# Retention, then two feed-forward layers, on one core: the first four chunks on two pairs of PSUM banks, with another order on VectorE and of the table loads

## The chip, the cores and the metric

The kernel runs on one core of a Trainium2 chip. The metric is the device time of one execution in microseconds (us), the median of several runs. One execution is also recorded by the hardware profiler; all views and rows below are of that one.

Engines, as the profile names them: PE is TensorE's matmul, PEld its weight load, DVE is VectorE, ACT is ScalarE, POOL is GpSimd, SP is SyncE, which issues most of the loads. Each engine runs its own instructions in order and waits for others by semaphores. A Q behind an engine's name (ACTq, SPq) is its sequencer, which issues DMAs.

## The reference

```python
def _attn_ref(q, k, v):                 # (4, 8, 768, 64) each
    gamma = 1.0 - 2.0 ** (-5.0 - np.arange(H, dtype=np.float32))
    for t in range(S):
        state = gamma[None, :, None, None] * state + np.einsum('bhd,bhe->bhde', k[:, :, t], v[:, :, t])
        y[:, :, t] = scale * np.einsum('bhd,bhde->bhe', q[:, :, t], state)

def _moe_ref(x, w_in, w_out):           # 3072 tokens, 512 -> 2048 -> 512
    h = x @ w_in
    g = np.where(h > 0.0, h, alpha * (np.exp(np.minimum(h, 0.0)) - 1.0))
    return g @ w_out

def _moe2_ref(x, w_in, w_out, g_ln):    # 512 -> 1024 -> 512
    h = x @ w_in
    sm = e / (np.sum(e, axis=-1, keepdims=True) + 1e-09)     # e = exp(h - max)
    solu = h * sm
    ln = (solu - mu) / np.sqrt(var + 1e-06) * g_ln
    return ln @ w_out
```

The three are chained: the output of the first, as 3072 tokens of 512 features, goes through the second and then the third.

## The kernel before

**Three stages.** The recurrence over time is done in chunks of C = 128 steps: 4 sequences of 6 chunks, 24 chunks, each with all 8 heads. Four chunks (CB = 4) make a block of 512 tokens, and there are NB = 6 blocks. Stage one turns chunks into attention outputs. Stage two is the feed-forward layer with 16 slices of 128 of its 2048 features per block: `up(j, f)` and `down(j, f)`. In it the chunks of the next block are worked in between, one per four slices. Stage three is the last layer, tile by tile of 128 tokens. All matrices are multiplied as a high and a low part, so each product is three matmuls, and ACT makes the high part and DVE the low part of everything.

**The opening.** This is where the change acts. Block 0 has no block before it to be worked into, so its four chunks run alone, ahead of `up(0, 0)`. For a chunk n the steps are:

- SP loads its tile in two halves of 512 KB (q and k transposed; then k and v). Before the others come the four small tables, which ACT issues: `v_decay` (4 KB), `q_decay` (256 KB), `causal` (64 KB), `state_decay` (2 KB).
- POOL: `decay_q(n)` (L326) multiplies q by `q_decay`, and `decay_v(n)` (L331) multiplies v by `v_decay`. It alternates the two, in the order of the chunks.
- TensorE: `scores(n)` (L394), 8 heads, fills two PSUM banks; it needs `decay_q(n)`. `key_values(n)` (L405) makes the chunk's addition to the state; it needs `decay_v(n)`. `values(n)` (L422 with the state, L425 with the masked scores) writes its output over the scores in the same two banks.
- DVE: `apply_mask(n)` (L589) copies the scores with the causal mask into `A[0]` or `A[1]` (A_68 and A_69 in the instruction lists below). `update_state(n)` (L610, or L613 and L615) makes the next state.
- `attended(n)`: ACT copies the output out of the banks as the high part `x_hi` (L776, semaphore `att_hi`), and then DVE subtracts this from the banks' content for the low part `x_lo` (L594, semaphore `att_lo`). After that the chunk's banks are free.

**Banks.** `att_bank(n)` gives the first of the two banks of a chunk. In the opening it is 2, 0, 4, 2 for chunks 0 to 3. Later chunks all have bank 2. The banks 6 and 7 belong to `key_values`. In stage two banks 0 and 1 are for `up`, 4 to 7 for `down`.

**What sets the order.** It is written out by hand for each engine. TensorE: `scores(0)`, then per chunk `key_values(n)`, `scores(n + 1)`, `values(n)` (L485 to L496). `scores(3)` waits for `att_lo` 1 (L383), since it takes chunk 0's banks. ACT alternates `attended(n)` and `split_hi`, which makes the high part of a block of weights; DVE's list in L622 to L641 has `split_lo` for their low parts among its chunk steps. `up(0, 0)` (L440, L441, then L446) starts when `att_hi` says that all four chunks have their high part. Ahead of `scores(0)` there are 14 matmuls on a tile of zeros (L484), which keep TensorE at work while the first tile is loaded.

Of the kernel before, what the change touches and what calls it, by code (L numbers as in the profile page):

```python
# [6 lines left out]
B, H, S, D = 4, 8, 768, 64  # L7
# [13 lines left out]
CB = TB // C  # L21
# [11 lines left out]
def build(nc, units, w1, w_in2, w_out2, g_ln, tables, x2_dram, out):  # L33
# [4 lines left out]
    with ctx:  # L38
# [31 lines left out]
        v_decay = place("v_decay", H, f32, CONST_AT + 32)  # L70
# [48 lines left out]
        ps = ctx.enter_context(nc.psum_tensor("ps", [P, 8 * 512], f32))[:, :].rearrange("p (b c) -> p b c", c=512)  # L119

        def att_bank(n):
            return (2, 0, 4, 2)[n] if n < CB else 2

        def ps_scores(n, h):
            return ps[:, att_bank(n) + h // HH, (h % HH) * C:(h % HH + 1) * C]
# [94 lines left out]
        def up_count(f):  # L220
            return 2 * f + 1
# [157 lines left out]
        def _(pe):  # L379

            def scores(n):
                pe.wait_ge(q_decayed, n + 1)
                if n == CB - 1:  # L383

                    pe.wait_ge(att_lo, 1)
                if n >= CB:

                    pe.wait_ge(att_lo, n)
                    pe.wait_ge(state_done, states(n))
                qt, kt = tile_of(n)[:, QT], tile_of(n)[:, KT]  # L390
                for hh in range(HH):
                    for h in (hh, HH + hh):
                        c = slice(hh * C, hh * C + C)
                        last = nc.tensor.matmul(ps_scores(n, h), kt[rows(h), c], qt[rows(h), c], start=True, stop=True)  # L394
                last.then_inc(scores_done, 1)

            def key_values(n):
                pe.wait_ge(v_decayed, n + 1)
                if 2 <= n < CB:
                    pe.wait_ge(state_done, states(n - 1))  # L400
                k, v = tile_of(n)[:, KN], tile_of(n)[:, VN]
                for hh in range(HH):
                    for h in (hh, HH + hh):
                        one = slice(h * D, (h + 1) * D)
                        last = nc.tensor.matmul(ps_kv(n)[rows(h), hh, :], k[:, one], v[:, one], start=True, stop=True,  # L405
                                                skip_group_check=True)
                last.then_inc(kv_done, 1)

            def values(n):
                c = n % NC  # L410
                qt, v = tile_of(n)[:, QT], tile_of(n)[:, VN]
                masked_scores = A[1 if n < CB and n % 2 else 0]
                pe.wait_ge(masked, n + 1)
                pe.wait_ge(v_decayed, n + 1)
                if c > 0:
                    pe.wait_ge(state_done, states(n))
                    for pair in range(2):
                        for half in range(2):
                            for odd in range(2):
                                h = HH * half + 2 * pair + odd  # L420
                                hh = h % HH
                                nc.tensor.matmul(ps_y(n, h), state[rows(h), n % 2, hh, :], qt[rows(h), hh * C:hh * C + C],  # L422
                                                 start=(pair == 0), stop=False, skip_group_check=True)
                for h in range(H):
                    last = nc.tensor.matmul(ps_y(n, h), v[:, h * D:(h + 1) * D], masked_scores[:, h, :],  # L425
                                            start=(c == 0 and h % HH < 2), stop=True, skip_group_check=True)
                last.then_inc(chunk_done, 1)
# [55 lines left out]
            for _ in range(WARM):  # L483
                nc.tensor.matmul(ps[:, 7, :], warm[:, 0:P], warm[:, :], start=True, stop=True)  # L484
            scores(0)  # L485
            key_values(0)
            scores(1)
            values(0)
            key_values(1)
            scores(2)  # L490
            values(1)
            key_values(2)
            scores(3)
            values(2)
            key_values(3)
            values(3)  # L496

            for j in range(NB):
                up(j, 0)
# [79 lines left out]
        def _(dve):  # L579

            def apply_mask(n):
                dve.wait_ge(scores_done, n + 1)
                before = n - 2 if n < CB else n - 1
                if before >= 0:

                    dve.wait_ge(chunk_done, before + 1)
                out_ = A[1 if n < CB and n % 2 else 0]
                scored = ps[:, att_bank(n):att_bank(n) + 2, :].rearrange("p b (h t) -> p (b h) t", h=HH)
                nc.vector.tensor_tensor(out_, scored, causal[:, :].unsqueeze(1).to_broadcast([P, H, C]), ALU.mult)\  # L589
                    .then_inc(masked, 1)  # L590

            def attended(n):
                dve.wait_ge(att_hi, n + 1)
                nc.vector.tensor_tensor(block_cols(x_lo, n), ps_y_all(n), block_cols(x_hi, n).bitcast(f32), ALU.subtract)\  # L594
                    .then_inc(att_lo, 1)

            def update_state(n):
                if n % NC == NC - 1:
                    return
                dve.wait_ge(kv_done, states(n + 1))  # L600
                if n > 0:

                    dve.wait_ge(chunk_done, n)
                if n >= CB:

                    dve.wait_ge(att_hi, n + 1)
                old, new = state[:, n % 2, :, :], state[:, (n + 1) % 2, :, :]
                decay = state_decay[:, :].unsqueeze(2).to_broadcast([P, HH, D])
                if n % NC == 0:
                    nc.vector.tensor_tensor(new, ps_kv(n), decay, ALU.mult).then_inc(state_done, 1)  # L610
                else:
                    dve.wait_ge(state_done, states(n))
                    nc.vector.tensor_tensor(state_sum, ps_kv(n), old, ALU.add).then_inc(state_summed, 1)  # L613
                    dve.wait_ge(state_summed, n - 2 * (n // NC))
                    nc.vector.tensor_tensor(new, state_sum, decay, ALU.mult).then_inc(state_done, 1)  # L615

            def split_lo(n, count):
                dve.wait_ge(w_hi_done, count)
                nc.vector.tensor_tensor(w_lo[:, n, :], w_raw[:, n, :], w_hi[:, n, :].bitcast(f32), ALU.subtract)\
                    .then_inc(w_lo_done, 1)  # L620
# [3 lines left out]
            dve.wait_ge(state_decay_in, 16)  # L624
            update_state(0)
            apply_mask(1)
            update_state(1)
            attended(0)
            apply_mask(2)
            update_state(2)  # L630
            apply_mask(3)
            attended(1)
            split_lo(0, up_count(0))
            attended(2)
            attended(3)
            split_lo(NF1, down_count(0))
# [118 lines left out]
        def _(act):  # L755
            for one_up in (y_sb_done, y_out[0], y_out[1]):
                act.sem_inc(one_up, 1)

            act.dma_start(v_decay[:, :], tables[:, T_VDEC:T_VDEC + H]).then_inc(v_decay_in, 16)
            act.dma_start(q_decay[:, :], tables[:, T_QDEC:T_QDEC + HH * C]).then_inc(q_decay_in, 16)  # L760
            act.dma_start(causal[:, :], tables[:, T_CAUSAL:T_CAUSAL + C]).then_inc(causal_in, 16)
            act.dma_start(state_decay[:, :], tables[:, T_SDEC:T_SDEC + HH]).then_inc(state_decay_in, 16)

            def split_hi(n):
# [170 lines left out]
```

## Time and profile before

| what | value |
|---|---|
| time, median of 3 runs | 904.7 us (904.67 to 904.89) |
| time of the profiled execution | 904.89 us |
| its span in the trace | 903.1 us |
| TensorE matmul busy | 894.6 us (99%) |
| VectorE / ScalarE / GpSimd busy | 408.0 / 304.1 / 117.3 us |
| mean granted clock of TensorE | 0.998 of full |
| HBM read / written | 44.44 / 12.58 MB |

The span is the time from the first to the last recorded instruction; the execution's own time is 1.79 us longer. A matmul's end is modelled, so two neighbouring ones overlap in the list: the distance of their starts tells the rate. The granted clock is the share of full speed that TensorE was allowed. In the rows below a bracket such as `[0.70 <-ACT x_hi L776]` says how long the engine was idle before the instruction and what ended that.

### The profile page before, as it was taken

The page shows a single profiled execution, that of the slowest core. Times are in us where ns is not written, and L with a number is a line of the kernel's source. Part 1 is how long each engine was busy: PE and PEld are TensorE (multiplying, and loading weights), DVE is VectorE, ACT ScalarE, POOL GpSimd, SP SyncE. Part 2 cuts the span into 40 slices and gives each one's busy share as a digit, 9 for nine tenths or more (in the row PEclk, how much of TensorE's full clock was granted, in tenths as well). Part 3 has the DMA queues.
Part 4 walks back from the last instruction along what each step waited for, and adds up shares of the span by engine and source line. Part 5 has one row for each costly group of instructions (what it writes and reads, how often), then busy time and mean ns, then how long its engine had stood idle before and what let it go on. Part 6 is the DMA issues. An engine that isn't in the chain of part 4 may idle for free.

```text
span 903.1 us, 12782 instructions
## 1 busy us (share of the span) xinstructions
PE 894.6 (99%) x5070; PEld 732.0 (81%) x5070; DVE 408.0 (45%) x712; ACT 304.1 (34%) x509; POOL 117.3 (13%) x106
## 2 busy tenths in 40 slices
PE   8999999999999999999999999999999999999998
PEld 6788888888888888888888888887888888888887
DVE  4765533332323333333423332266765655566563
ACT  2645332322423233332423333353232223322322
POOL 4211101110201111110200000122211111111110
PEclk9999999999999999999999999999999999999999
DMA  9901131110410131110400020312111111111100
GB/s 349 406 18 40 47 94 47 48 48 1 140 32 16 47 94 47 47 47 1 140 1 1 1 70 1 120 63 75 43 38 35 46 46 46 46 46 46 46 35 36
DMA packets 33675, 57.65 MB, mean 64 GB/s; under 512 B 3040, under 2 KB 15584, under 8 KB 33632
## 3 DMA queue, kind: packets, MB, share of 16 engines
q1 hardware_dynamic: 33056, 56.70, 18.2%
q8 instruction: 32, 0.52, 0.2%
q10 hardware_dynamic: 576, 0.33, 0.1%
q14 instruction: 11, 0.09, 0.0%
HBM read 44.44 MB, written 12.58 MB: 63 GB/s over the span
## 4 chain that ended last, share of the span: by engine, by line
PE 96%; DVE 1%; issue 1%; POOL 0%; DMA 0%; ACT 0%; DVEq 0%; POOLq 0%; ACTq 0%
PE ps L462 11%; PE ps L466 10%; PE ps L463 10%; PE ps L440 10%; PE ps L441 10%; PE ps L446 10%; PE ps L535 5%; PE ps L537 5%; PE ps L536 5%; PE ps L477 4%; PE ps L479 4%; PE ps L478 4%; PE ps L394 3%; PE ps L425 3%; PE ps L523 2%
## 5 line engine op out<-in xcount | busy, mean ns | idle before, releaser
L462 PE MATMUL ps<-g_hi,w_hi 128*128 128x512 f32 x384 | 154.0, 401 | 0.0
L651 DVE TENSOR_TENSOR g_lo<-e,g_hi 128x512 fp32r<-128x512 f32 x96 | 74.9, 780 | 170.3 <-ACT g_hi L803 170.1
L440 PE MATMUL ps<-x_hi,w_hi 128*128 128x512 f32 x384 | 149.5, 389 | 0.7 <-ACT x_hi L776 0.7
L466 PE MATMUL ps<-g_lo,w_hi 128*128 128x512 f32 x384 | 149.9, 390 | 0.0
L463 PE MATMUL ps<-g_hi,w_lo 128*128 128x512 f32 x384 | 149.6, 390 | 0.0
L441 PE MATMUL ps<-x_hi,w_lo 128*128 128x512 f32 x384 | 149.4, 389 | 0.0
L646 DVE SCALAR_TENSOR_TENSOR e<-e,ps 128x512 f32<-128x512 f32 x96 | 65.7, 684 | 141.0 <-ACT e L797 141.0
L803 ACT ACTIVATE g_hi<-e 128x512 fp32r<-128x512 f32 x96 | 60.7, 632 | 198.4 <-PE ps L466 187.1
L795 ACT ACTIVATE e<-ps 128x512 f32<-128x512 f32 x96 | 57.3, 597 | 149.6 <-PE ps L446 148.8
L446 PE MATMUL ps<-x_lo,w_hi 128*128 128x512 f32 x384 | 102.6, 389 | 0.0
L462 PEld LDWEIGHTS ps<-g_hi,w_hi 128*128 128x128 f32 x384 | 72.0, 188 | 17.9 <-issue 0.7
L440 PEld LDWEIGHTS ps<-x_hi,w_hi 128*128 128x128 f32 x384 | 72.1, 188 | 15.9 <-ACT x_hi L776 0.9
L466 PEld LDWEIGHTS ps<-g_lo,w_hi 128*128 128x128 f32 x384 | 72.1, 188 | 15.4
L441 PEld LDWEIGHTS ps<-x_hi,w_lo 128*128 128x128 f32 x384 | 72.1, 188 | 15.0
L446 PEld LDWEIGHTS ps<-x_lo,w_hi 128*128 128x128 f32 x384 | 72.1, 188 | 15.0
L463 PEld LDWEIGHTS ps<-g_hi,w_lo 128*128 128x128 f32 x384 | 72.1, 188 | 14.0
L326 POOL TENSOR_TENSOR tiles<-tiles,q_decay 128x512 f32<-128x512 f32 x23 | 31.8, 1384 | 385.9 <-DMA tiles<-units_dram 379.5
L535 PE MATMUL ps<-w_hi,n_hi 128*128 128x512 f32 x192 | 75.0, 391 | 0.1
L537 PE MATMUL ps<-w_hi,n_lo 128*128 128x512 f32 x192 | 74.9, 390 | 0.0
L536 PE MATMUL ps<-w_lo,n_hi 128*128 128x512 f32 x192 | 74.7, 389 | 0.0
L477 PE MATMUL ps<-w_hi,x_hi 128*128 128x512 f32 x184 | 73.7, 400 | 0.0
L479 PE MATMUL ps<-w_hi,x_lo 128*128 128x512 f32 x184 | 71.8, 390 | 0.0
(82 smaller groups left out, 1067.8 us busy)
## 6 DMA issues: line engine op xcount, KB each, us to landing
tiles<-units_dram SPq DMA_DIRECT2D x46, 512.0 KB, 4.7
w_raw<-w_dram SPq DMA_DIRECT2D x32, 256.0 KB, 9.5
x_between<-x SPq DMA_DIRECT2D x24, 256.0 KB, 2.7
x_tile<-x_between SPq DMA_DIRECT2D x24, 256.0 KB, 2.7
out_dram<-y_sb SPq DMA_DIRECT2D x24, 256.0 KB, 2.0
w_raw<-w_in_dram SPq DMA_DIRECT2D x4, 512.0 KB, 5.0
w_raw<-w_out_dram SPq DMA_DIRECT2D x4, 512.0 KB, 3.4
tile<-units_dram SPq DMA_DIRECT2D x2, 512.0 KB, 10.1
```

Source lines behind the costliest of these rows:

```text
L440: nc.tensor.matmul(bank, hi, x_hi[:, j % 2, k, :], start=(k == 0), stop=False)
L441: nc.tensor.matmul(bank, lo, x_hi[:, j % 2, k, :], start=False, stop=False)
L446: last = nc.tensor.matmul(bank, hi, x_lo[:, j % 2, k, :], start=False, stop=(k == KD - 1))
L462: nc.tensor.matmul(ps[:, 4 + m, :], hi, g_hi[:, f % 2, :], start=(f == 0), stop=False)
L463: nc.tensor.matmul(ps[:, 4 + m, :], lo, g_hi[:, f % 2, :], start=False, stop=False)
L466: last = nc.tensor.matmul(ps[:, 4 + m, :], hi, g_lo[:, f % 2, :], start=False, stop=(f == NF1 - 1))
L477: nc.tensor.matmul(bank, x_h[:, k, :], hi, start=(k == 0), stop=False)
L479: last = nc.tensor.matmul(bank, x_l[:, k, :], hi, start=False, stop=(k == KD - 1))
L535: nc.tensor.matmul(bank, n_hi[:, par, f, :], hi, start=(f == 0), stop=False)
L536: nc.tensor.matmul(bank, n_hi[:, par, f, :], lo, start=False, stop=False)
L537: last = nc.tensor.matmul(bank, n_lo[:, par, f, :], hi, start=False, stop=(f == NF2 - 1))
L651: nc.vector.tensor_tensor(g_lo[:, f % 2, :], e[:, f % 2, :], g_hi[:, f % 2, :].bitcast(f32), ALU.subtract)\
```

## The change

Four edits, all of them in the opening. (1) The chunks 0 to 3 have the bank pairs 2, 4, 2, 4 in place of 2, 0, 4, 2, so in the opening each chunk takes the pair of the chunk two before. Therefore `scores(2)` and `scores(3)` wait until `att_lo` has 1 and 2. (2) The TensorE order of the opening is written as a loop. (3) On DVE `attended(0)` goes ahead of `update_state(1)`, and `attended(1)` and `split_lo(0)` go ahead of `update_state(2)` and `apply_mask(3)`. (4) ACT issues the table `v_decay` third in place of first.

```diff
@@ -119,7 +119,7 @@
         ps = ctx.enter_context(nc.psum_tensor("ps", [P, 8 * 512], f32))[:, :].rearrange("p (b c) -> p b c", c=512)
 
         def att_bank(n):
-            return (2, 0, 4, 2)[n] if n < CB else 2
+            return 4 if n < CB and n % 2 else 2
 
         def ps_scores(n, h):
             return ps[:, att_bank(n) + h // HH, (h % HH) * C:(h % HH + 1) * C]
@@ -380,12 +380,11 @@
 
             def scores(n):
                 pe.wait_ge(q_decayed, n + 1)
-                if n == CB - 1:
-
-                    pe.wait_ge(att_lo, 1)
+                before = n - 2 if n < CB else n - 1
+                if before >= 0:
+
+                    pe.wait_ge(att_lo, before + 1)
                 if n >= CB:
-
-                    pe.wait_ge(att_lo, n)
                     pe.wait_ge(state_done, states(n))
                 qt, kt = tile_of(n)[:, QT], tile_of(n)[:, KT]
                 for hh in range(HH):
@@ -483,17 +482,11 @@
             for _ in range(WARM):
                 nc.tensor.matmul(ps[:, 7, :], warm[:, 0:P], warm[:, :], start=True, stop=True)
             scores(0)
-            key_values(0)
-            scores(1)
-            values(0)
-            key_values(1)
-            scores(2)
-            values(1)
-            key_values(2)
-            scores(3)
-            values(2)
-            key_values(3)
-            values(3)
+            for n in range(CB):
+                key_values(n)
+                if n + 1 < CB:
+                    scores(n + 1)
+                values(n)
 
             for j in range(NB):
                 up(j, 0)
@@ -624,13 +617,13 @@
             dve.wait_ge(state_decay_in, 16)
             update_state(0)
             apply_mask(1)
+            attended(0)
             update_state(1)
-            attended(0)
             apply_mask(2)
+            attended(1)
+            split_lo(0, up_count(0))
             update_state(2)
             apply_mask(3)
-            attended(1)
-            split_lo(0, up_count(0))
             attended(2)
             attended(3)
             split_lo(NF1, down_count(0))
@@ -756,9 +749,9 @@
             for one_up in (y_sb_done, y_out[0], y_out[1]):
                 act.sem_inc(one_up, 1)
 
-            act.dma_start(v_decay[:, :], tables[:, T_VDEC:T_VDEC + H]).then_inc(v_decay_in, 16)
             act.dma_start(q_decay[:, :], tables[:, T_QDEC:T_QDEC + HH * C]).then_inc(q_decay_in, 16)
             act.dma_start(causal[:, :], tables[:, T_CAUSAL:T_CAUSAL + C]).then_inc(causal_in, 16)
+            act.dma_start(v_decay[:, :], tables[:, T_VDEC:T_VDEC + H]).then_inc(v_decay_in, 16)
             act.dma_start(state_decay[:, :], tables[:, T_SDEC:T_SDEC + HH]).then_inc(state_decay_in, 16)
 
             def split_hi(n):
```

TensorE in the opening, from `key_values(1)` on, before and then after. The names in it: `tiles` and `tile_67` are the chunks' inputs, `ps` is PSUM.

```order
L405 MATMUL ps<-tiles 64x64 [waits v_decayed]
L405 MATMUL ps<-tiles 64x64 x7
L394 MATMUL ps<-tiles 128x128 [waits q_decayed]
L394 MATMUL ps<-tiles 128x128 x7
L422 MATMUL ps<-tiles,state 64x128 [waits state_done,v_decayed,masked]
```

```order
L404 MATMUL ps<-tiles 64x64 [waits v_decayed]
L404 MATMUL ps<-tiles 64x64 x7
L393 MATMUL ps<-tiles 128x128 [waits att_lo,q_decayed]
L393 MATMUL ps<-tiles 128x128 x7
L421 MATMUL ps<-tiles,state 64x128 [waits state_done,v_decayed,masked]
```

Nothing has moved on TensorE; `scores(2)` has a second wait, `att_lo`. The lines of the changed kernel have other numbers (one lower here, seven lower on DVE and ACT). `scores(3)` has that wait in both, for a higher count after.

DVE in the opening, from the mask of chunk 1 to the mask of chunk 3, before and then after:

```order
L589 TENSOR_TENSOR A_69<-ps,causal 128x1024 [waits scores_done]
L613 TENSOR_TENSOR state_sum<-ps,state 128x256 [waits state_done,chunk_done,kv_done]
L615 TENSOR_TENSOR state<-state_sum,state_decay 128x256 [waits state_summed]
L594 TENSOR_TENSOR x_lo<-ps,x_hi 128x4x128 [waits att_hi]
L589 TENSOR_TENSOR A_68<-ps,causal 128x1024 [waits chunk_done,scores_done]
L613 TENSOR_TENSOR state_sum<-ps,state 128x256 [waits state_done,chunk_done,kv_done]
L615 TENSOR_TENSOR state<-state_sum,state_decay 128x256 [waits state_summed]
L589 TENSOR_TENSOR A_69<-ps,causal 128x1024 [waits chunk_done,scores_done]
```

```order
L582 TENSOR_TENSOR A_69<-ps,causal 128x1024 [waits scores_done]
L587 TENSOR_TENSOR x_lo<-ps,x_hi 128x4x128 [waits att_hi]
L606 TENSOR_TENSOR state_sum<-ps,state 128x256 [waits state_done,chunk_done,kv_done]
L608 TENSOR_TENSOR state<-state_sum,state_decay 128x256 [waits state_summed]
L582 TENSOR_TENSOR A_68<-ps,causal 128x1024 [waits chunk_done,scores_done]
L587 TENSOR_TENSOR x_lo<-ps,x_hi 128x4x128 [waits att_hi]
L612 TENSOR_TENSOR w_lo<-w_raw,w_hi 128x512 [waits w_hi_done]
L606 TENSOR_TENSOR state_sum<-ps,state 128x256 [waits state_done,chunk_done,kv_done]
L608 TENSOR_TENSOR state<-state_sum,state_decay 128x256 [waits state_summed]
L582 TENSOR_TENSOR A_69<-ps,causal 128x1024 [waits chunk_done,scores_done]
```

The subtraction `x_lo` of chunk 0 now stands ahead of the two steps of the state of chunk 1, and that of chunk 1 together with the first `w_lo` ahead of those of chunk 2.

ACT's first four instructions that issue DMAs, before and then after, with what follows them:

```order
L759 DMA v_decay<-tables_dram 128x8
L760 DMA q_decay<-tables_dram 128x512
L761 DMA causal<-tables_dram 128x128
L762 DMA state_decay<-tables_dram 128x4
L776 ACT_TABLE_LOAD
```

```order
L752 DMA q_decay<-tables_dram 128x512
L753 DMA causal<-tables_dram 128x128
L754 DMA v_decay<-tables_dram 128x8
L755 DMA state_decay<-tables_dram 128x4
L769 ACT_TABLE_LOAD
```

`v_decay` has moved from the first to the third place of the queue.

## Rows read from the trace of the kernel before

**Rows 1.** The page, part 4: shares of the chain that ended last, by engine.

```profile
PE 96%; DVE 1%; issue 1%; POOL 0%; DMA 0%; ACT 0%; DVEq 0%; POOLq 0%; ACTq 0%
```

**Rows 2.** The chain of the first 30 us: start us, duration us, what.

```profile
13.34 1.02 PE ps L425 x16
...
17.54 0.46 PE ps L405 x16
...
21.78 1.05 PE ps L425 x16
...
22.85 0.61 ACT x_hi L776
```

**Rows 3.** Timeline of TensorE: start us, duration us, work [idle before it].

```profile
8.95 1.49 PE L394 MATMUL ps<-tiles 64*128 64x128 f32 x16 [2.03 <-POOL tiles L326]
...
11.42 1.92 PE L394 MATMUL ps<-tiles 64*128 64x128 f32 x16
13.27 1.09 PE L425 MATMUL ps<-A,tiles 128*64 128x128 f32 x16
...
14.76 1.16 PE L394 MATMUL ps<-tiles 64*128 64x128 f32 x16
15.85 0.67 PE L422 MATMUL ps<-tiles,state 64*64 64x128 f32 x16
...
17.93 1.16 PE L394 MATMUL ps<-tile 64*128 64x128 f32 x16
...
23.50 0.50 PE L440 MATMUL ps<-x_hi,w_hi 128*128 128x512 f32 x1 [0.70 <-ACT x_hi L776]
23.84 0.40 PE L441 MATMUL ps<-x_hi,w_lo 128*128 128x512 f32 x1
24.08 0.40 PE L440 MATMUL ps<-x_hi,w_hi 128*128 128x512 f32 x1
```

**Rows 4.** Timeline of VectorE, opening.

```profile
13.39 1.23 DVE L589 TENSOR_TENSOR A<-ps,causal 128x1024 f32<-128x1024 f32 x1 [1.28 <-PE ps L394]
...
23.48 0.69 DVE L594 TENSOR_TENSOR x_lo<-ps,x_hi 128x512 fp32r<-128x512 f32 x1 [1.32 <-ACT x_hi L776]
```

**Rows 5.** Timeline of all engines, start: when four loads are issued.

```profile
0.96 0.39 ACTq L759 DMA_DIRECT2D v_decay<-tables_dram  x1
...
1.39 0.45 ACTq L760 DMA_DIRECT2D q_decay<-tables_dram  x1
1.67 0.43 SPq L236 DMA_DIRECT2D tiles<-units_dram  x1
...
1.86 0.45 ACTq L761 DMA_DIRECT2D causal<-tables_dram  x1
```

**Rows 6.** DMA issues: KB each, us from issue to landing.

```profile
q_decay<-tables_dram ACTq DMA_DIRECT2D x1, 256.0 KB, 6.2
causal<-tables_dram ACTq DMA_DIRECT2D x1, 64.0 KB, 7.3
...
v_decay<-tables_dram ACTq DMA_DIRECT2D x1, 4.0 KB, 4.1
...
tiles<-units_dram SPq DMA_DIRECT2D x1, 512.0 KB, 7.0
```

**Rows 7.** Timeline of GpSimd, opening.

```profile
7.63 1.26 POOL L326 TENSOR_TENSOR tiles<-tiles,q_decay 128x512 f32<-128x512 f32 x1 [6.33 <-DMA q_decay<-tables_dram]
8.85 1.05 POOL L331 TENSOR_TENSOR tiles<-tiles,v_decay 128x512 f32<-128x512 f32 x1
9.85 1.27 POOL L326 TENSOR_TENSOR tiles<-tiles,q_decay 128x512 f32<-128x512 f32 x1
```

**Rows 8.** Stretches: busy us (PE, PEld, DVE, ACT, POOL), clock, DMA share, GB/s.

```profile
9.00:9.50 0.50, 0.50 (x9) 0.50 (x11) 0.00 (x0) 0.00 (x0) 0.50 (x1) 1.00 1.06 321
...
10.00:13.00 3.00, 3.00 (x35) 2.66 (x34) 1.56 (x2) 0.00 (x0) 3.00 (x3) 0.50 1.02 399
...
13.50:20.00 6.50, 6.50 (x134) 5.78 (x132) 5.87 (x8) 2.23 (x4) 3.32 (x3) 1.00 1.04 407
```

## The prediction, made before the changed kernel ran

> **What bounds the kernel now.** I read the page's chain first: 96% of what ended last is TensorE [rows 1]. So only time that TensorE loses counts, and I ask where the edits touch its path. They all act in the opening, the four chunks of block 0 before the first `up`. Next, the chain of the first 30 us: chunk 0's `values` ends at 13.34 + 1.02 = 14.36 us, chunk 1's at 17.54 us, where L405 begins, chunk 3's at 21.78 + 1.05 = 22.83 us, and the first `up` waits for ACT's copy of it [rows 2]. The timeline of TensorE has two idle times from 7 us on: 2.03 us for the first decayed q, and 0.70 us before `up` [rows 3]. Between them a next group is ready at once: TensorE is the bound there too. Behind `up(0, 0)` at 23.50 us no edit follows, and TensorE is the chain, so a later `up(0, 0)` moves the end by the same amount. The weights go on loading by SP's own order, and a later TensorE gives them more time.
>
> The profiled execution is 904.89 us (span 903.1 and 1.79 around it); the median of the three runs is 904.70. I work out a difference and put it on the median.
>
> **The banks and the new waits (a cost).** Before, chunks 1 and 2 have banks of their own: `scores(2)` starts at 14.76 us, right behind `key_values(1)`, and `scores(3)` at 17.93 us right behind `key_values(2)` [rows 3]. With two pairs, `scores(2)` needs the pair of chunk 0, which is free when both `attended` of chunk 0 have read it. The path from the end of a `values` to there, from chunk 3, whose copy and subtraction have no other work ahead of them: chain end 22.83, ACT L776 from 22.85, DVE L594 from 23.48 for 0.69, ends 24.17 [rows 2, 4]. With 0.04 from there to a matmul (as from ACT's end at 22.85 + 0.61 = 23.46 to 23.50 [rows 2, 3]) that is 24.21 - 22.83 = 1.38 us. Under it lies only `key_values(1)`, which filled what was a 0.40 us step from 14.36 to 14.76 [rows 2, 3]. Stall one: 1.38 - 0.40 = 0.98 us. For `scores(3)`, which before waited only for chunk 0's `att_lo`, long there: 17.93 - 17.54 = 0.39, so stall two is 0.99 us. A restart costs a little more: at 23.50 us the first step from matmul to matmul is 0.34 us, the next 0.24 [rows 3], so 0.10 each, 0.20. Sum 2.17 us, or 1.97 if the 64-row matmuls restart free.
>
> **The DVE order.** `attended(0)` now stands ahead of `update_state(1)`, and `attended(1)` and the first `split_lo` ahead of `update_state(2)`. Without this the stalls would be longer. Is DVE free for `attended(0)`? The mask of chunk 1 starts 0.05 us behind the scores (13.39 to 13.34) and lasts 1.23 [rows 2, 4]; the scores' end plus `values(0)` (1.02) plus ACT's copy (0.65) is later, at 1.67. Yes, by 0.39 us. What is queued behind: `update_state(1)` needs two operations half as wide as L594's, at most 0.69 us each, while `values(2)`, which wants that state, is over 3 us away. `mask(3)` waits behind `attended(1)`, `split_lo(0)` and `update_state(2)`. Counted from the end of `scores(1)`, `attended(1)` ends at about 6.6 us (the two stalls and 1.62 us per `values` laid end to end); three operations of at most 0.69 and the mask's 1.23 end by 9.9, and `values(3)` wants the mask at 9.8 to 9.9. So the cover is small but there even at that upper bound: the edit costs nothing, 0.1 us at worst. The loop in place of the written-out list issues the same TensorE groups in the same order: 0.
>
> **The table loads (both signs).** On ACT's queue the first three tables landed in order: `v_decay` 0.96 + 4.1 = 5.06, `q_decay` 1.39 + 6.2 = 7.59, `causal` 1.86 + 7.3 = 9.16 [rows 5, 6]. The sizes are 4, 256 and 64 KB, yet the steps behind the first are 2.5 and 1.6 us: each costs its place among SP's 512 KB loads more than its bytes. If the first 256 KB take the first place, `q_decay` lands about 1 us (2.5 less the 1.6 of a place) behind 5.06, at 6.1 (5.1 to 7.2), not 7.6. But `v_decay` is now third, and the first three together still end near 9.16 (8.6 to 9.6): I take that row, since the three transfers are the same. GpSimd runs in order: `decay_q(0)` 6.1 to 7.4, then it waits until 9.2 for the 4 KB table, `decay_v(0)` 1.05 to 10.25, `decay_q(1)` 1.27 to 11.52 [rows 7]. So `scores(0)` starts 1.5 us earlier, at 7.45, and `key_values(0)` near 10.3, but `scores(1)` near 11.58: 0.16 us later than the 11.42 of before [rows 3]. What was a gain at the head is given back behind it. The `causal` table lands earlier than now and its mask is not near it.
>
> The Trainium skill, page "DMA: Bandwidth & Descriptors", section "Anatomy of one DMA", gives a fixed cost of about 2.0 us for a transfer plus its bytes at 436 GB/s (measured there on GpSimd's path). By it 4 KB issued at 1.86 us would be there at 3.9 us and GpSimd would never wait for it; that is the rival N below. The trace doesn't agree: 4.1 us for the same 4 KB at the head of its queue, and 7.3 us for 64 KB in third place [rows 6].
>
> **The clock.** The granted clock is full (2.4 GHz) up to 9.5 us, half (1.2 GHz) from 10 to 13 us, and full again from 13.5 us [rows 8]. It fell after TensorE had stood for 2.03 us and worked again for about 0.6 us [rows 3], and rose after it had worked without a gap. At half level lay `key_values(0)` and nearly all of `scores(1)`, whose step to `values(0)` is 13.27 - 11.42 = 1.85 us against 1.09 for the same group at 14.76 (to 15.85) [rows 3]. In the changed kernel TensorE has done 1.1 us more by then but again stands for about 1.8 us and 0.8 us. I cannot compute what the chip decides. I take the low stretch as it was (in `scores(1)`), because TensorE is still idle for most of the time between 6.9 and 11.6 us. Then `values(0)` starts at 13.27 + 0.16.
>
> **Sum.** 0.16 + 0.98 + 0.99 + 0.20 = 2.33 us over the median: 907.0 us. A measurement of this kernel can tell about 0.2%, 1.8 us, from no change: the bounds are 902.9 and 906.5.
>
> **Rivals.**
> H, the clock holds: enough work comes early that it never falls. `scores(1)` takes 1.09, `values(0)` starts at 12.67, 0.60 us earlier than now; -0.60 + 2.17 = +1.57, 906.3 us. For it: `scores(0)` at 7.45 follows the warm-up after 0.5 us. Against: the gap just moves behind `scores(0)`.
> L, the clock stays low longer, or falls later and covers `values(0)`, `key_values(1)` and part of `scores(2)`. At half level the 1.02 and 0.46 us of the first two double: +1.5 us, less what the stall hides of it. With the front as in H that comes to about 907.2, with the front as forecast to about 908.3. For it: the two stalls put idle time into what was an unbroken stretch.
> N, `v_decay` isn't late (the other side, not slower). If it lands by 7.4 us, GpSimd goes on at once: `decay_v(0)` to 8.45, `decay_q(1)` when its tile is there (1.67 + 7.0 = 8.7 [rows 5, 6]), to about 10.12. `scores(1)` starts at 10.17, 1.25 us earlier than now, and with a full clock ends 2.01 us earlier; against 2.17 of stalls that is 904.9 us, no difference. With a low clock it is 905.9. It decides below a landing of 8.1 us or so, from which point the front gains more than 0.5 us. Against it: the landings in order of issue.
> F, faster by more than 1.8 us: N, and both stalls hidden. Nothing covers them on TensorE.
>
> **How the numbers follow.** Forecast as worked out, with the milder form of L (906.7 to 907.5): 0.46. H 0.23. Harder L (907.9 to 908.6) 0.14. N 0.14, mostly 904.9 to 905.9. F 0.03. Slower by over 0.2%: nearly all of the forecast (0.43), all of the harder L (0.14), a quarter of H (0.06): 0.63. Faster 0.03. Same 0.34. The range, which leaves out half of N, the upper half of L's hard form and F, is 905.4 to 908.3; with 0.1 to 0.4 us for the cover of `mask(3)` and the landing of `v_decay` it needs no more.
>
> **What would show it.** Right: TensorE stands for about 1 us ahead of `scores(2)` and again ahead of `scores(3)`, each ended by DVE's `x_lo`; GpSimd stands between `decay_q(0)` and `decay_v(0)`, ended by `v_decay`; `scores(0)` near 7.5 us; the first `up` near 25.8 us; from there on the same distances as now. Wrong: stalls under 0.5 us each (then DVE or ACT is quicker than chunk 3's rows say); GpSimd going on at once (N); a granted clock without the low stretch (H) or with a longer one (L); or a wait named behind the first `up` that wasn't there. The forecast is wrong in sign if the first `up` starts before 23.5 us.

## The result, and the profile after

| | before | changed |
|---|---|---|
| median, 5 runs each | 904.7 us (904.41 to 904.89) | 909.56 us (908.45 to 910.17) |
| ratio, 95% interval | | 1.0055 (1.0044 to 1.0067) |
| profiled execution, its span | 904.89, 903.1 us | 909.62, 907.8 us |

The changed kernel is slower by 4.9 us, where 2.3 were forecast: the direction was right, and the time lies above the range. The five executions spread over 1.7 us, those of before over 0.5; in 14 executions in all the changed kernel took 908.39 to 911.29 us.

The chain of the first 34 us of the changed kernel (start, duration, what) answers to [rows 2]:

```profile
9.83 1.04 POOL tiles L331
...
12.15 1.42 PE ps L393 x16
13.57 1.93 PE ps L424 x16
...
15.52 0.61 ACT x_hi L769
...
16.15 0.70 DVE x_lo L587
...
16.98 1.16 PE ps L393 x16
...
21.05 1.63 DVE w_lo L612
...
23.40 1.23 DVE A L582
...
30.37 2.65 DVE w_lo L612 x3
...
33.67 0.50 PE ps L439
```

Read it against the prediction. The chain no longer starts at a q: it comes over `decay_v(0)` on GpSimd (L331), which waits for `v_decay`. `scores(1)` (L393) starts at 12.15 us, `values(0)` (L424) at 13.57 takes 1.93 us, and then the two stalls come as forecast: ACT's `x_hi`, DVE's `x_lo`, the next `scores` at 16.98 and again at 21.28. New is that between the second stall and the first `up` (27.06 us) a weight subtraction on DVE (L612, 1.63 us) and the mask it holds up (L582) are on the chain; and behind the first `up` DVE is on it once more, until the third `up` (L439) starts at 33.67 us. By engine, the page says of the whole chain, against [rows 1], 94% in place of 96% for TensorE and 2% in place of 1% for VectorE:

```profile
PE 94%; DVE 2%; issue 1%; DMA 1%; POOL 1%; ACT 0%; ACTq 0%; DVEq 0%; POOLq 0%
```

TensorE's waits from 6 to 60 us (total, times, longest):

```profile
PE ps L404 <- POOL tiles L331: 2.2, 1, 2.2
PE ps L393 <- DVE x_lo L587: 1.7, 2, 1.1
...
PE ps L439 <- DVE e L639: 0.9, 1, 0.9
PE ps L439 <- ACT x_hi L769: 0.7, 1, 0.7
```

The last but one of these isn't in the kernel before: 0.88 us for DVE's `e`, behind the first `up`. The third `up` (`up(0, 2)`) starts here in the kernel before (TensorE, timeline):

```profile
29.11 0.39 PE L440 MATMUL ps<-x_hi,w_hi 128*128 128x512 f32 x1
```

and here in the changed one:

```profile
33.67 0.50 PE L439 MATMUL ps<-x_hi,w_hi 128*128 128x512 f32 x1 [0.88 <-DVE e L639]
```

From the first `up` to the third it is 29.11 - 23.50 = 5.61 us before ([rows 3] for the first) and 33.67 - 27.06 = 6.61 after. With that the loss of the profiled execution can be cut up along TensorE's starts in the timeline (where `values(0)` starts at 13.50, a little ahead of the chain's 13.57):

| step | before | after | later by |
|---|---|---|---|
| to `values(0)` | 13.27 | 13.50 | 0.23 |
| `values(0)` to `scores(2)` | 1.49 | 3.48 | 1.99 |
| `scores(2)` to `scores(3)` | 3.17 | 4.30 | 1.13 |
| `scores(3)` to the first `up` | 5.57 | 5.78 | 0.21 |
| first `up` to third | 5.61 | 6.61 | 1.00 |

The sum is 4.56 of the 4.73 us between the two profiled executions. The second row holds the first stall (0.66 us of idle time, ended by DVE's `x_lo`) and the slow clock of `values(0)` and `key_values(1)`; the third holds the second stall, 1.05 us idle.

Two of the tables (KB, us from issue to landing) answer to [rows 6]; they are issued at 0.96 and 1.87 us:

```profile
q_decay<-tables_dram ACTq DMA_DIRECT2D x1, 256.0 KB, 5.3
...
v_decay<-tables_dram ACTq DMA_DIRECT2D x1, 4.0 KB, 7.9
```

`q_decay` lands at about 6.25, `v_decay` at about 9.76 us, in third place. And the granted clock, with the columns of [rows 8]:

```profile
9.00:12.50 3.50, 1.04 (x22) 0.90 (x24) 1.54 (x2) 0.00 (x0) 2.67 (x3) 1.00 1.00 347
13.00:16.00 3.00, 3.00 (x36) 2.78 (x36) 1.22 (x1) 0.48 (x1) 3.00 (x4) 0.50 1.03 416
17.00:20.00 3.00, 3.00 (x62) 2.71 (x64) 2.04 (x3) 0.19 (x1) 0.56 (x1) 1.00 1.05 417
```

It is full until 12.5 us, half from 13 to 16 us and full again. The low stretch lies about 3 us later than in before, over `values(0)` and `key_values(1)` instead of `key_values(0)` and `scores(1)`.

### The profile page after: what moved, and what is told of

Same layout as the page of the kernel before. It is cut to its first block, busy times and chain, and to the rows that moved or that the text cites. A ratio compares the mean times of both kernels' runs of the same rounds, so it can differ in the third digit from the quotient of the medians.

```text
span 907.8 us, 12783 instructions
## 1 busy us (share of the span) xinstructions
PE 895.2 (99%) x5070; PEld 732.0 (81%) x5070; DVE 410.8 (45%) x712; ACT 304.0 (33%) x509; POOL 115.8 (13%) x106
## 4 chain that ended last, share of the span: by engine, by line
PE 94%; DVE 2%; issue 1%; DMA 1%; POOL 1%; ACT 0%; ACTq 0%; DVEq 0%; POOLq 0%
PE ps L461 11%; PE ps L465 10%; PE ps L462 10%; PE ps L439 9%; PE ps L440 9%; PE ps L445 9%; PE ps L528 5%; PE ps L530 5%; PE ps L529 5%; PE ps L476 4%; PE ps L478 4%; PE ps L477 4%; PE ps L424 3%; PE ps L393 3%; PE ps L516 2%; PE ps L421 1%
## 5 line engine op out<-in xcount | busy, mean ns | idle before, releaser
L439 PE MATMUL ps<-x_hi,w_hi 128*128 128x512 f32 x384 | 149.6, 390 | 1.6 <-DVE e L639 0.9
L439 PEld LDWEIGHTS ps<-x_hi,w_hi 128*128 128x128 f32 x384 | 72.1, 188 | 17.1 <-DVE e L639 1.3
```

The costliest lines, as they stand in the source:

```text
L439: nc.tensor.matmul(bank, hi, x_hi[:, j % 2, k, :], start=(k == 0), stop=False)
```

## The experiments

Three letters name the parts of the change: B is the two bank pairs with their waits, D the order on VectorE, T the table order. B can't be had with the old order on VectorE, since there `attended(1)` stands behind `mask(3)`, which would then wait for it in a circle. The executions of one kernel differ in their mean granted clock; where an execution is said to be at full clock, that mean is 0.999 or 1.000. Where a profile was taken, the low stretch lies in the opening. Before, at full clock, lies at 903.8 to 904.5 us (904.1 in the middle), at 0.998 at 904.4 to 905.2; one execution at 0.996 took 908.26.

**D alone**, `D_order_only`:

```diff
-            update_state(1)
             attended(0)
+            update_state(1)
             apply_mask(2)
-            update_state(2)
-            apply_mask(3)
             attended(1)
             split_lo(0, up_count(0))
+            update_state(2)
+            apply_mask(3)
```

> The kernel before with the new VectorE order alone (banks and tables as before). Theory A (the parts add up from waits in the opening): attended(0) goes ahead of the state of chunk 1, nothing on TensorE waits for either early, so 904.7 us, within 0.3. Rival B (the order itself costs, because update_state(2) and mask(3) stand behind a weight subtraction): first up later by 0.3 to 1 us, 905.0 to 905.7.

Measured: 905.11 us against 904.43, ratio 1.0002 (0.9991 to 1.0012); at full clock 904.14 to 904.56, else 905.0 to 906.2. No difference that the interval tells, though the trace has a small one. TensorE, and then DVE:

```profile
21.52 0.67 PE L422 MATMUL ps<-tile,state 64*64 64x128 f32 x16 [0.31 <-DVE A L589]
```

```profile
18.85 0.68 DVE L619 TENSOR_TENSOR w_lo<-w_raw,w_hi 128x512 fp32r<-128x512 f32 x1
...
20.25 1.22 DVE L589 TENSOR_TENSOR A<-ps,causal 128x1024 f32<-128x1024 f32 x1
```

`mask(3)` (L589) starts at 20.25 us, behind the subtraction at 18.85 and the state, though its scores ended at about 19.1; so `values(3)` starts at 21.52, 0.31 us after TensorE could have gone on. The prediction had worked out the cover for the changed kernel, where the stalls give VectorE more time; here there are none, so this wait doesn't contradict it.

**T alone**, `T_tables_only`, and **D and T without B**, `DT_banks_back`:

```diff
-            act.dma_start(v_decay[:, :], tables[:, T_VDEC:T_VDEC + H]).then_inc(v_decay_in, 16)
             act.dma_start(q_decay[:, :], ...)
             act.dma_start(causal[:, :], ...)
+            act.dma_start(v_decay[:, :], tables[:, T_VDEC:T_VDEC + H]).then_inc(v_decay_in, 16)
```

> The kernel before with v_decay issued third and nothing else. Theory A: v_decay lands near 9.76 us as in the changed kernel, scores(1) starts near 12.15 instead of 11.42; the granted clock then falls later and lies over values(0) and key_values(1): first up 0.7 to 1.6 us later than 23.5, and 905.4 to 906.5 in all, with runs that differ by up to 2 us according to where the low stretch falls. Rival B (most of the loss is the tables and the clock): 907 or more. Rival C (only the banks cost): 904.7.

> The changed kernel with the four banks of before back (chunks 1 and 2 on their own pairs), new VectorE order and new table order kept. Theory A: the two stalls ahead of scores(2) and scores(3) are gone, first up near 24.6 to 25.1, no wait for VectorE behind it: 905.5 to 906.7. Rival B (tables and clock carry the loss): over 907.5.

Measured: T 906.82 us (904.47 to 908.99), ratio 1.0024 (1.0011 to 1.0037). DT 907.26 us (906.75 to 909.51), ratio 1.0038 (1.0024 to 1.0052). Both medians lie between theory A and rival B, above what the waits in the opening add up to. T's ten executions fall into groups: 904.47 to 904.77 at full clock, 905.4 to 906.9 at 0.998, 908.4 to 909.0 at 0.996. So moving one 4 KB table costs 0.4 to over 4 us in the same program, and the time follows the clock. The profiled execution of T (908.42 us, clock 0.996) shows how a low clock comes to cost so much. Its first `up` starts at 25.44 us, 1.94 us later than before. Its third starts here:

```profile
32.52 0.50 PE L440 MATMUL ps<-x_hi,w_hi 128*128 128x512 f32 x1 [1.35 <-DVE e L646]
```

That is 7.08 us behind the first, 1.47 more than before, although T changes nothing on VectorE and adds no bank wait. The two parts, 3.41 us, are nearly all of the 3.53 us between the two executions. DT has the same in small: 1.55 us by the first `up`, and 6.23 us from there to the third. What the second part is comes below.

**B and D without T**, `BD_v_first`, the changed kernel with `v_decay` first:

> The changed kernel with v_decay issued first again; two bank pairs and new VectorE order kept. Theory A: GpSimd does not wait, scores(1) at 11.42 as before, two stalls of 1.0 to 1.1 us, first up near 25.7; behind it VectorE's weight subtractions meet GpSimd's decays of chunks 4 and 5 and run longer, up(0, 2) waits up to 0.9 us: 906.9 to 907.9. Rival B (tables and clock carry the loss): under 906.2.

Measured: 907.82 us (906.58 to 909.02), ratio 1.0039 (1.0026 to 1.0051); three executions at full clock took 906.6 to 907.0, three at 0.998 took 908.7 to 909.0. The profiled execution was at full clock, and shows the stalls clean (TensorE, timeline):

```profile
13.23 0.64 PE L404 MATMUL ps<-tiles 128*64 128x64 f32 x16
14.91 1.16 PE L393 MATMUL ps<-tiles 64*128 64x128 f32 x16 [1.05 <-DVE x_lo L587]
...
17.53 0.63 PE L404 MATMUL ps<-tiles 128*64 128x64 f32 x16
19.21 1.16 PE L393 MATMUL ps<-tile 64*128 64x128 f32 x16 [1.05 <-DVE x_lo L587]
...
24.78 0.50 PE L439 MATMUL ps<-x_hi,w_hi 128*128 128x512 f32 x1 [0.70 <-ACT x_hi L769]
...
31.02 0.50 PE L439 MATMUL ps<-x_hi,w_hi 128*128 128x512 f32 x1 [0.50 <-DVE e L639]
```

From the start of `key_values` (L404) to the next `scores` it is 1.68 us both times, against 0.57 us for the same step before (14.19 to 14.76 us): 1.11 us each, of which the rows name 1.05 as idle. These are the two stalls of the forecast. The first `up` comes at 24.78 us. But the third comes 6.24 us behind it, with an idle 0.50 us for DVE, where `D_order_only` (23.91 to 29.50) has 5.59.

**Why does DVE come late?** In this part of the changed kernel the weight subtractions (L612) that last longer than 0.68 us (one) or 1.89 us (three in a row) lie beside GpSimd's decays of chunks 4 and 5:

```profile
21.05 1.63 DVE L612 TENSOR_TENSOR w_lo<-w_raw,w_hi 128x512 fp32r<-128x512 f32 x1
...
30.29 2.73 DVE L612 TENSOR_TENSOR w_lo<-w_raw,w_hi 128x512 fp32r<-128x512 f32 x3
```

```profile
20.87 1.26 POOL L326 TENSOR_TENSOR tiles<-tiles,q_decay 128x512 f32<-128x512 f32 x1 [3.31 <-DMA tiles<-units_dram]
...
28.48 1.60 POOL L326 TENSOR_TENSOR tiles<-tiles,q_decay 128x512 f32<-128x512 f32 x1 [3.98 <-DMA tiles<-units_dram]
30.05 1.22 POOL L331 TENSOR_TENSOR tiles<-tiles,v_decay 128x512 f32<-128x512 f32 x1
```

The subtraction from 21.05 lasts 1.63 us; GpSimd's decay runs from 20.87 to 22.13, and 22.13 plus 0.55 is the subtraction's end. This is what the Trainium skill, page "SBUF — State Buffer", section "SBUF: two separate sides", describes: VectorE with two SBUF inputs and GpSimd take a shared port pair in turn, whoever starts first for its whole instruction. The end 0.55 us behind the decay agrees with that. The trace alone doesn't prove it, since the weight loads run then too. Two experiments take the meeting away. `BDT_small_45` is the changed kernel with almost nothing for GpSimd to do in those chunks:

```diff
+                w = 1 if n in (4, 5) else HH * C
-                nc.gpsimd.tensor_tensor(qt, qt, q_decay[:, :], ALU.mult).then_inc(q_decayed, 1)
+                nc.gpsimd.tensor_tensor(qt[:, 0:w], qt[:, 0:w], q_decay[:, 0:w], ALU.mult).then_inc(q_decayed, 1)
```

(and `decay_v` likewise, to one column of each head).

> The changed kernel in which GpSimd's decays of chunks 4 and 5 work on one column in place of all (this leaves out part of the decay of these two chunks), so that they last 0.1 to 0.2 us each. Theory A (VectorE's subtractions with two inputs in SBUF stand while a GpSimd decay runs, and this lengthens the way to up(0, 2)): the 1.63 us subtraction ahead of mask(3) takes 0.7, the three ahead of the first elu take 1.9 in place of 2.7, no wait for VectorE ahead of up(0, 2); 0.9 to 1.4 us less than the changed kernel: 908.1 to 908.7 where that has 909.5. Rival B (VectorE is late by its own list, whatever GpSimd does): within 0.3 us of the changed kernel.

Measured: 907.92 us (906.75 to 910.55), 1.6 us below the changed kernel. Since the clock spreads both, compare at equal clock: at full clock 906.75 (one execution) against 908.39 to 908.45, at 0.998 two at 907.79 and 907.92 against 909.4 to 910.2. Both give about 1.7 us. Its subtractions:

```profile
20.62 0.68 DVE L614 TENSOR_TENSOR w_lo<-w_raw,w_hi 128x512 fp32r<-128x512 f32 x1
...
28.99 1.89 DVE L614 TENSOR_TENSOR w_lo<-w_raw,w_hi 128x512 fp32r<-128x512 f32 x3
```

0.68 and 1.89 us, and the third `up` follows the first by 5.60 us again (26.41 to 32.01). The test is in the three: the single one lies clear of the decay of chunk 4, which starts at 22.29 us here. Rival B fell: with the same loads and the same list VectorE isn't late.

**Mask first**, `BDT_mask_first`: in the changed kernel `split_lo(0)` goes behind `mask(3)`.

> The changed kernel with the first weight subtraction, split_lo(0), moved behind mask(3) on VectorE. Theory A: the 0.3 us for which values(3) waits for its mask goes, and nothing else: first up 0.3 to 0.5 us earlier, 909.1 to 909.3. Rival B: as the subtraction now meets another decay, the gain is given back behind the first up: 909.5.

Measured: 908.4 us (908.32 to 909.84, four runs), ratio 1.0049 (1.0032 to 1.0065). The executions at full clock, 908.32 to 908.44, equal those of the changed kernel at full clock, 908.39 to 908.45. That is neither theory A nor rival B, and it can't decide between them: the next experiment shows that at full clock the subtraction in its old place takes 0.68 us and no mask is waited for, so there was nothing to gain. The wait for the mask, 0.2 us, belongs to the profiled execution of the changed kernel, where the opening is later. The fourth execution, at 0.996, took 909.84 us, against 909.8 and 910.4 of the changed kernel at that clock.

**Filling the hole**, `BDT_fill`: eight warm-up matmuls ahead of `key_values(0)` in the changed kernel.

```diff
             scores(0)
+            for _ in range(8):
+                nc.tensor.matmul(ps[:, 7, :], warm[:, 0:P], warm[:, :], start=True, stop=True)
             for n in range(CB):
                 key_values(n)
```

> The changed kernel with eight more warm-up matmuls of 512 columns between scores(0) and key_values(0), where TensorE stands for 2.2 us. Theory A (part of the loss is the low clock, which falls because TensorE has stood): the clock stays full through values(0) and key_values(1), first up about 1.1 us earlier than at 27.06, and the runs lie near the best of the changed kernel: 908.2 to 908.6 with little spread. Rival B (the clock is not set by that hole): it falls all the same and the eight matmuls cost up to 1 us more: 909.5 to 910.5.

Measured: 908.42 us, and four runs within 908.33 to 908.64. The clock:

```profile
9.00:16.00 7.00, 4.88 (x75) 3.67 (x75) 3.51 (x6) 1.11 (x2) 6.33 (x6) 1.00 1.02 373
```

It never falls, and the four executions equal those of the changed kernel at full clock. So 1.1 us of the changed kernel's median is the low clock, and filling the time in which TensorE stood keeps it from falling. What remains is 4.3 us above before at full clock (904.1), in which DVE meets GpSimd in full. TensorE's waits, then DVE, then GpSimd:

```profile
PE ps L393 <- DVE x_lo L589: 2.1, 2, 1.1
...
PE ps L439 <- DVE e L641: 1.3, 1, 1.3
```

```profile
28.13 3.84 DVE L614 TENSOR_TENSOR w_lo<-w_raw,w_hi 128x512 fp32r<-128x512 f32 x3
```

```profile
28.49 1.48 POOL L326 TENSOR_TENSOR tiles<-tiles,q_decay 128x512 f32<-128x512 f32 x1 [4.04 <-DMA tiles<-units_dram]
29.94 1.49 POOL L331 TENSOR_TENSOR tiles<-tiles,v_decay 128x512 f32<-128x512 f32 x1
```

The three subtractions take 3.84 us, and the third `up` follows the first by 7.08 us (25.55 to 32.63). **T with the fill**, `T_fill`, is the kernel before with T and the same eight matmuls:

> The kernel before with v_decay third (T_tables_only: 904.5 to 909.0, median 906.8) and eight filling matmuls between scores(0) and key_values(0). Theory A (what the table order alone costs is nearly all low clock, from the hole behind scores(0)): full clock in every run and 904.4 to 904.9 with a spread of a few tenths. Rival B (the table order costs by the later decay_q(1)): 906 or more.

Measured: 904.49 us, ten runs within 904.34 to 904.86, ratio 1.0003 (0.9994 to 1.0012), where T alone had 906.82. Theory A: at full clock the table order costs 0.4 us in the kernel before. Its first `up` starts at 23.19 us and the third 5.60 us later, so without the low clock VectorE isn't late either. With the two stalls present the same edit costs more: from `BD_v_first` to `BDT_fill`, both profiled at full clock, the first `up` moves from 24.78 to 25.55 us, 0.77 later, and the step to the third grows from 6.24 to 7.08. The parts of this change don't simply add.

**Holding GpSimd**, `BDT_fill_hold`, does all the work and only orders the two engines:

```diff
             for n in range(1, NCH):
+                if n == 5:
+                    pool.wait_ge(w_lo_done, 6)
                 decay_q(n)
```

> The changed kernel with the eight filling matmuls (as in BDT_fill, 908.4 us) and one more wait: GpSimd starts the decays of chunk 5 only when VectorE has done its sixth weight subtraction. All work is done. Theory A (the two engines take turns on something that a subtraction with two SBUF inputs and a GpSimd decay both need): the three subtractions ahead of the first elu take 1.9 in place of 3.84 us, the 1.35 us wait of up(0, 2) goes, 907.0 to 907.2. Rival B (something else makes VectorE slow at that time, such as the loads): unchanged, 908.4.

Measured: 906.76 us (906.67 to 907.0, eight runs), ratio 1.0026 (1.0016 to 1.0037), 1.66 us below `BDT_fill` by one wait. DVE, then GpSimd:

```profile
27.96 1.89 DVE L616 TENSOR_TENSOR w_lo<-w_raw,w_hi 128x512 fp32r<-128x512 f32 x3
...
30.37 1.41 DVE L616 TENSOR_TENSOR w_lo<-w_raw,w_hi 128x512 fp32r<-128x512 f32 x1
```

```profile
29.93 1.30 POOL L326 TENSOR_TENSOR tiles<-tiles,q_decay 128x512 f32<-128x512 f32 x1 [5.91 <-DVE w_lo L616]
```

The three take 1.89 us. The decay starts at 29.93, and now the subtraction at 30.37 lasts 1.41 us and ends 0.55 us behind the decay (31.23): the meeting isn't gone but lies where nobody on the path waits for it. The third `up` follows the first by 5.60 us (25.38 to 30.98): 1.48 of the 1.66 us, and the first `up` came 0.17 earlier in that execution.

**A version that beats both.** If each table costs its place, both of GpSimd's tables belong ahead: `q_v_causal` is the kernel before with the order q, v, causal.

```diff
-            act.dma_start(v_decay[:, :], tables[:, T_VDEC:T_VDEC + H]).then_inc(v_decay_in, 16)
             act.dma_start(q_decay[:, :], ...)
+            act.dma_start(v_decay[:, :], tables[:, T_VDEC:T_VDEC + H]).then_inc(v_decay_in, 16)
             act.dma_start(causal[:, :], ...)
```

> The kernel before with the tables in the order q_decay, v_decay, causal, state_decay, nothing else. Theory A (each transfer on ScalarE's queue costs its place, so what counts is that both tables that GpSimd needs are ahead): q_decay lands near 5.9 to 6.3, v_decay near 7.5 to 8.3, scores(1) at 10.2 to 10.6 in place of 11.42; first up 22.4 to 23.0 with a full clock: 903.4 to 904.3. Rival B (the clock falls in the new hole and takes it back): 904.7 to 905.5. Rival C (an earlier TensorE meets the late tile of chunk 3 or a weight load): 904.7.

> The same kernel as q_v_causal, in more rounds, to tell whether it is faster than the kernel before. Theory A (q and v tables first brings the first up forward by 1.0 us at equal clock, and keeps the clock from falling): 903.9 to 904.2 against 904.4 to 904.7, ratio 0.9995 with runs closer together. Rival B: no difference.

Measured: 904.1 us (ten runs) and 904.12 us (eleven runs), ratios 0.9998 (0.9988 to 1.0007) and 0.9996 (0.9987 to 1.0005): no difference that the interval tells, and none against the executions of before at full clock (904.1). The clock was full in every run. Yet the opening is much shorter. Tables, then TensorE:

```profile
q_decay<-tables_dram ACTq DMA_DIRECT2D x1, 256.0 KB, 4.8
...
v_decay<-tables_dram ACTq DMA_DIRECT2D x1, 4.0 KB, 6.5
```

```profile
10.27 1.16 PE L394 MATMUL ps<-tiles 64*128 64x128 f32 x16 [0.54 <-POOL tiles L326]
...
21.67 0.50 PE L440 MATMUL ps<-x_hi,w_hi 128*128 128x512 f32 x1 [0.70 <-ACT x_hi L776]
...
28.00 0.50 PE L440 MATMUL ps<-x_hi,w_hi 128*128 128x512 f32 x1 [0.16 <-DVE e L646]
```

`scores(1)` starts at 10.27 us and the first `up` at 21.67, 1.8 us earlier than [rows 3] has it. Part of that is the clock, which stayed full here; no profile of before at full clock says how large a part. But the third `up` comes 6.33 us behind the first in place of 5.6: 0.73 us is given back there, with two subtractions at 22.25 us that take 2.49 us beside the decay of chunk 4. So the hold was put to it as well, `q_v_causal_hold` (`if n == 4: pool.wait_ge(w_lo_done, 5)`):

> The kernel before with the tables in the order q, v, causal (904.1), and GpSimd's decays of chunk 4 held until VectorE has done its fifth weight subtraction. Theory A: the two subtractions at 22 us take 1.28 in place of 2.49, the 0.16 us wait of up(0, 2) goes, 903.9 to 904.1. Rival B: the held decays meet the subtractions of the first elus, and down(0, 0) waits: 904.1 to 904.6.

Measured: 903.27 us (903.05 to 903.51, ten runs), ratio 0.9987 (0.9978 to 0.9997): faster than the kernel before by 1.1 us, 0.8 against its executions at full clock. The interval is only just clear of 1. It is 0.85 us below `q_v_causal`, more than expected. The two subtractions:

```profile
22.49 1.29 DVE L621 TENSOR_TENSOR w_lo<-w_raw,w_hi 128x512 fp32r<-128x512 f32 x2
```

1.29 us in place of 2.49. The held decays now lie beside the subtractions behind the first `elu` (the function between `up` and `down`), and nothing on TensorE waits for these. The third `up` is 5.58 us behind the first (21.90 to 27.48), so the 0.73 us is gone. The expectation had counted the named idle time of 0.16 us alone; the second `up`, which also waits for a subtraction, had been late too (24.80 to 21.67 is 3.13 us, against 2.85 with the hold). TensorE's waits from 6 to 40 us are then those of the tables and of the first `up`:

```profile
PE ps L396 <- POOL tiles L326: 1.3, 2, 0.8
...
PE ps L442 <- ACT x_hi L778: 0.7, 1, 0.7
```

## Why the prediction was right and wrong

The step that failed is "Behind `up(0, 0)` at 23.50 us no edit follows, and TensorE is the chain, so a later `up(0, 0)` moves the end by the same amount". The runs showed in its place that a later `up(0, 0)` moves VectorE's subtractions into GpSimd's decays, and the third `up` comes up to 1.5 us later still.

At full clock the difference is 908.4 - 904.1 = 4.3 us. With GpSimd held it is 906.76 - 904.1 = 2.66, which the two stalls (2.22) and the table order (0.4, from `T_fill`) account for. The meeting of VectorE and GpSimd is the other 1.65. The medians differ by 4.86 since the low clock puts 1.16 us on the changed kernel and 0.6 on the one before. The forecast had 2.17 for the stalls, 0.16 for the table order, and nothing for the meeting or for a clock that falls elsewhere. That its sign was right rests on the stalls, which it had right.

**The bank waits: right.** 0.98 and 0.99 us were forecast with 0.20 for restarts, sum 2.17; the trace at full clock has 1.11 each, sum 2.22.

**The table order: the mechanism right, the size near.** The step "the first three together still end near 9.16" held in kind: `q_decay` landed at 6.25 (6.1 forecast), GpSimd stood 2.28 us for `v_decay`, and `key_values(0)` and `scores(1)` were late. `v_decay` landed at 9.76 in the profiled execution, just outside the stated 8.6 to 9.6; `scores(1)` started at 12.15 in place of 11.58, and at full clock the order costs 0.4 us where 0.16 was forecast. Rival N, and with it what was worked out from a fixed cost per transfer, is out: in third place the 4 KB took 7.5 to 7.9 us in eight kernels. (N's own sums are off: a tile at 8.7 us and 1.27 of work end at 9.97, not 10.12, and 904.7 + 2.17 - 1.25 is 905.6, not 905.9. The forecast doesn't use them.)

**The clock: wrong, and it was a rival.** "I take the low stretch as it was (in `scores(1)`)" failed. In the profiled execution it fell about 3 us later and lay over `values(0)`, as L had it. Of the 14 executions three had a mean clock of 1.000 and three of only 0.994; where it was low in those no trace shows. `BDT_fill` shows that filling the hole behind `scores(0)` keeps it full, and what the low clock adds to the changed kernel's median, 1.1 us; before has 0.6 us of the kind in its own. L was priced at up to 908.3 since it was added to stalls alone.

**"A later `up(0, 0)` moves the end by the same amount": wrong, and the main error.** The step from the first to the third `up` grew from 5.61 to 6.61 us in the profiled execution, and at full clock to 7.08 (`BDT_fill`). The prediction looked at what TensorE waited for before, and found nothing; it didn't ask which work on other engines keeps its own time. GpSimd's decays of chunks 4 and 5 hang on SP's loads, which came at nearly the same time in all kernels (decay of chunk 5 from 27.8 to 28.5 us on). A later opening moves VectorE's subtractions into them. In the profile of before the weight subtractions met them only behind the first `elu`, where nothing waited. This is 1.65 us, by `BDT_fill_hold` and by `BDT_small_45`. The same meeting is the second part of what T cost at low clock.

**VectorE's order: wrong in the bound, nearly right in the cost.** The "three operations of at most 0.69" took the duration of one that ran alone as an upper end. The trace of before, from which it was read, already had longer ones. VectorE, then GpSimd:

```profile
15.33 0.89 DVE L615 TENSOR_TENSOR state<-state_sum,state_decay 128x256 f32<-128x256 f32 x1
...
28.50 1.30 DVE L619 TENSOR_TENSOR w_lo<-w_raw,w_hi 128x512 fp32r<-128x512 f32 x1
```

```profile
14.67 1.28 POOL L326 TENSOR_TENSOR tile<-tile,q_decay 128x512 f32<-128x512 f32 x1 [0.31 <-DMA tile<-units_dram]
```

The half-wide step of the state takes 0.42 us elsewhere and 0.89 beside this decay; 0.68 us for a subtraction became 1.30 beside the decay of chunk 5. Asking why would have led to the meeting and its price. In the profiled execution of the changed kernel the subtraction took 1.63 us and `values(3)` started 0.2 us late. At full clock (`BD_v_first`, `BDT_fill`) the cover held, and the step from `scores(3)` to the first `up` is 5.57 us, as before.

What stays open: why the clock falls in one execution of a program and not in the next; the runs show only that less standing time keeps it up. And that VectorE and GpSimd share a port is the Trainium skill's account: the runs show that they hinder each other, that it goes when they are kept apart, and that the weight loads aren't its cause.

## What to carry to other kernels

A delay at the start isn't carried through unchanged, even where one engine is busy for the rest: ask which transfers and which engines keep their own time, and what the delayed work will now meet. An operation's duration is that of the company it had; bound it by its longest case, and for VectorE with two SBUF inputs look at what GpSimd does in those microseconds. A small transfer costs its place in the queue, so issue first what a strictly ordered engine wants first, all of it and not only the largest.

## What the hardware showed that was not expected

A subtraction of 128x512 on VectorE with both inputs in SBUF takes 0.68 us alone and 0.9 to 1.8 us when it starts while GpSimd's decay is under way; it then ends about 0.55 us behind that. One with an input in PSUM kept its 0.68 us (`x_lo` at 16.15 us in before, inside the decay from 15.91 to 17.13). Three in a row took 1.89, 2.7, 3.0 and 3.84 us. GpSimd's decays in turn took 1.27 and 1.04 us alone and up to 1.86 and 1.5 us then.

A table of 4 KB took 4.1 us to land at the head of its queue, 6.5 to 6.7 in second and 7.5 to 7.9 us in third place, beside loads of 512 KB.

Executions of one unchanged program differed by 4.5 us (T alone), with mean granted clocks from 1.000 down to 0.996. The low clock costs twice: by its own stretch in the opening, and by what the delayed VectorE then meets. With eight matmuls in the idle time all 22 executions (three kernels) were at full clock, and those of one kernel differed by 0.5 us at most.
